# The first normalisation of a fused attention and feed-forward kernel, reordered on all engines

## The reference

```
attention:   4 batches, 8 heads, 576 positions, head width 64
             softmax(q k' / 8 + mask) v       heads 0-3: the last 32 positions
                                              heads 4-7: every 32nd position
feed-forward: rms = sqrt(mean(x*x, axis=-1) + 1e-6);  xn = x / rms * rms_g
             out = (silu(xn @ w_gate) * (xn @ w_val)) @ w_out      width 1536
experts:     8 experts of width 1024, each token goes to the one with the largest logit
             relu(x @ w1[e]) @ w2[e], scaled by the softmax gate
```

## Time and profile before

| what | us |
|---|---|
| median of 3 runs | 873.07 |
| lowest and highest | 871.36 and 874.25 |
| span of the profiled execution | 870.5 |
| TensorE busy | 857.1 (98%) |
| VectorE busy | 520.7 (60%) |
| ScalarE busy | 374.4 (43%) |
| GpSimd busy | 328.4 (38%) |

### The profile page before, as it was taken

One profiled execution on the slowest core, in us unless ns is written; L12 is line 12 of the kernel. 1 busy time (PEld: TensorE's weight loads), 2 busy tenths in 40 slices (PEclk: granted clock), 3 DMA queues, 4 the chain that ended last, 5 costly groups with the idle time before them and its releaser, 6 DMA issues.

```text
span 870.5 us, 15612 instructions
## 1 busy us (share of the span) xinstructions
PE 857.1 (98%) x5233; PEld 736.4 (85%) x5242; DVE 520.7 (60%) x1401; ACT 374.4 (43%) x945; POOL 328.4 (38%) x372
## 2 busy tenths in 40 slices
PE   8999999999999999999999999999999999999997
PEld 5678898888888888899999999988888888888885
DVE  6985555333453335449778763883877457666663
ACT  6966313545464455443321132243356235554442
POOL 3736762344323443356335333170043221222211
PEclk9999999999999999999999999999999999999999
DMA  9983212212223210242121121526265645555531
GB/s 191 289 212 88 61 48 65 84 55 78 53 60 112 52 38 27 71 157 74 42 93 61 61 73 37 210 81 254 97 205 206 241 144 191 184 213 182 192 128 39
DMA packets 77517, 103.40 MB, mean 119 GB/s; under 512 B 38973, under 2 KB 43069, under 8 KB 77312
## 3 DMA queue, kind: packets, MB, share of 16 engines
q1 hardware_dynamic: 73760, 91.16, 33.9%
q0 software_dynamic: 3680, 11.28, 3.7%
HBM read 92.98 MB, written 10.22 MB: 119 GB/s over the span
## 4 chain that ended last, share of the span: by engine, by line
PE 89%; DVE 8%; issue 1%; ACT 1%; POOL 1%; DMA 1%; SPq 0%; DVEq 0%; POOLq 0%; ACTq 0%
PE ps L1243 32%; PE ps L1282 16%; PE ps L1805 13%; PE ps L1790 13%; PE ps L1174 3%; PE ps L1203 2%; PE ps L1815 2%; PE ps L1184 2%; PE ps L1150 2%; PE ps L660 1%; DVE sm L1520 1%; DVE w_lo L2041 1%; DMA qk<-in_k 1%; PE ps L1312 1%; DVE h_lo L1600 1%
## 5 line engine op out<-in xcount | busy, mean ns | idle before, releaser
L1035 POOL TENSOR_TENSOR sm<-sm,rinv 72x288 f32<-72x288 f32 (+1 forms) x51 | 45.5, 893 | 174.2 <-DVE rinv L1531 174.1
L1067 POOL TENSOR_TENSOR out_lo<-out_raw,out_hi 128x512 fp32r<-128x512 f32 x72 | 101.8, 1414 | 5.8
L1589 DVE SCALAR_TENSOR_TENSOR h<-h,ps 128x384 f32<-128x384 f32 x72 | 39.8, 553 | 104.2 <-ACT h L1437 103.3
L1243 PE MATMUL ps<-x_hi,val_hi 128*128 128x384 f32 x288 | 101.1, 351 | 0.0
L1243 PE MATMUL ps<-x_hi,gate_hi 128*128 128x384 f32 x288 | 100.5, 349 | 0.4 <-DVE h L1589 0.4
L1065 POOL CAST out_hi<-out_raw 128x512 fp32r<-128x512 f32 x72 | 50.0, 694 | 135.0 <-DMA out_raw<-in_moe_w_out 135.0
L1441 ACT ACTIVATE h_hi<-h 128x384 fp32r<-128x384 f32 x72 | 37.8, 525 | 138.7 <-DVE h L1595 138.7
L1243 PE MATMUL ps<-x_hi,gate_lo 128*128 128x384 f32 x288 | 97.1, 337 | 0.0
L1243 PE MATMUL ps<-x_hi,val_lo 128*128 128x384 f32 x288 | 96.6, 336 | 0.0
L1243 PE MATMUL ps<-x_lo,val_hi 128*128 128x384 f32 x288 | 96.5, 335 | 0.0
L1243 PE MATMUL ps<-x_lo,gate_hi 128*128 128x384 f32 x288 | 93.9, 336 | 0.0
(11 more groups left out here) (278 smaller groups left out, 1947.5 us busy)
## 6 DMA issues: line engine op xcount, KB each, us to landing
w_raw<-in_moe_w SPq DMA_DIRECT2D x72, 512.0 KB, 4.9
out_raw<-in_moe_w_out SPq DMA_DIRECT2D x72, 256.0 KB, 2.6
x_rows<-y_tiles SPq DMA_DIRECT2D x18, 256.0 KB, 2.7
early_w_raw<-in_moe_w SPq DMA_DIRECT2D x8, 512.0 KB, 7.6
gate_raw<-in_moe_w_gate SPq DMA_DIRECT2D x4, 768.0 KB, 9.1
val_raw<-in_moe_w_val SPq DMA_DIRECT2D x4, 768.0 KB, 10.5
qk<-in_q SPq DMA_DIRECT2D x8, 288.0 KB
qk<-in_k SPq DMA_DIRECT2D x8, 288.0 KB
```

What stands on the lines that cost most here:

```text
L1035: pool.tensor_tensor(s3, s3, rinv[0:n, i, :].unsqueeze(2).to_broadcast([n, 4, c]), ALU.mult).then_inc(s_no, 1)
L1067: pool.tensor_tensor(ol[i][:, :], o_raw[i][:, :], oh[i][:, :].bitcast(f32), ALU.subtract).then_inc(s_ol, 1)
L1243: mm = pe.matmul(ps[:, bank, 0:CH], w[:, i, kk, cols], x[:, kk, :], start=(m == 0), stop=(m == n - 1))
L1589: dve.scalar_tensor_tensor(out=hf[n % 2][:, :], in0=hf[n % 2][:, :], scalar=1.0, in1=ps[:, 0, 0:CH], op0=ALU.add, op1=ALU.mult).then_inc(s ...
```

## The change

The parts are:

1. In GpSimd's loop the normalises of a tick now go ahead of its squares, and the last square of chunk 0 is at tick 15 instead of 16. It is followed by a multiplication of the gain by 0.375, for which GpSimd waits for the load of the gain.
2. Quarter 0 of val is rounded at tick 17 instead of 13, and GpSimd itself then subtracts its two halves (`first_val_lo`).
3. The sums of chunk 0 are split: those of `nr` at tick 16, those of `sq` at tick 17, into two banks, added by VectorE. The mean's factor is in the column of constants `share`.
4. The roots have eight linked operations after the variance instead of eleven and no diagonals: one bit trick, one Newton step and one step of higher order, whose factor 0.375 is in the gain. They are spread by three transposes of a root column read as broadcast. This holds for all chunks.
5. In VectorE's loop the inverts now go ahead of the roots, and normalise and split of x ahead of the mask passes of tick 19.
6. ScalarE splits x in pieces of one, one and two, around the evacuations of tick 19. The exps of groups 18 and 19 move from ticks 18 and 20 to ticks 20 and 21.
7. `first_block` issues block 0 of chunk 0 as hi terms of gate, hi terms of val, lo terms of gate, lo terms of val, one to a tick. The values of tick 20 go behind its first part.
8. The matmuls of constants are 2, 3, 2 and 2 in ticks 16 to 19 instead of 3, 3, 2 and 4. The root spread of chunk 0 goes ahead of those of tick 18.

```diff
-EXPS = {j: SCORE[j] + (0 if j < HEAD - 1 else 1) for j in range(G)}
-INVERT = {j: SCORE[j] + (1 if j < HEAD - 1 else 2 if j < HEAD else 3) for j in range(G)}
+EXPS = {j: SCORE[j] + (0 if j < HEAD - 2 else 2 if j < HEAD else 1) for j in range(G)}
+INVERT = {j: SCORE[j] + (1 if j < HEAD - 2 else 2 if j < HEAD else 3) for j in range(G)}
-SQUARES = {(0, 2): 8, (0, 3): 12, (0, 0): 14, (0, 1): 16}
+SQUARES = {(0, 2): 8, (0, 3): 12, (0, 0): 14, (0, 1): 15}
-SPLIT_V = {0: 13, 1: at(0, 1, 1), 2: at(0, 4, 1), 3: at(0, 7, 1)}
+SPLIT_V = {0: 17, 1: at(0, 1, 1), 2: at(0, 4, 1), 3: at(0, 7, 1)}
...
         def front_pool(pool):
...
             pool.memset(ones[:, :], 1.0).then_inc(s_cst, 1)
+            pool.memset(share[:, :], 1.0 / DM).then_inc(s_cst, 1)
...
                 pool.tensor_tensor(sq[:, :], x, x, ALU.mult).then_inc(s_sq, 1)
                 if kk == ORDER[-1] and c == 0:
+                    pool.wait_ge(s_gain, 16)
+                    pool.tensor_scalar(rms_gain[:, :], rms_gain[:, :], 0.375, None, ALU.mult).then_inc(s_gain38, 1)
                     return
...
+            def first_val_lo():
+                pool.wait_ge(s_wh, SPLIT_NO[1, 0] + 1)
+                for ks in (slice(0, KT // 2), slice(KT // 2, KT)):
+                    pool.tensor_tensor(vl[:, 0, ks, :], v_raw[:, 0, ks, :], vh[:, 0, ks, :].bitcast(f32),
+                                       ALU.subtract).then_inc(s_fv, 1)
...
             for s in range(TICKS):
+                for j in NORM_AT.get(s, []):
+                    normalise(j)
                 if s < EARLY:
                     for c, kk in SQUARES_AT.get(s, []):
                         square(c, kk)
-                for j in NORM_AT.get(s, []):
-                    normalise(j)
                 for val, i in SPLIT_AT.get(s, []):
                     w_hi(val, i)
+                    if (val, i) == (1, 0):
+                        first_val_lo()
...
         def front_pe(pe):
...
-            def sum_squares(c):
-
-                if c:
-                    bank_7_free(("ss", c))
-                else:
-                    pe.wait_ge(s_cst, 3)
-                    pe.wait_ge(s_qe, TURNED_QK[EARLY])
-                pe.wait_ge(s_sq, sq_steps(c + 1))
+            def sum_squares(of, bank, done=s_ssq):
+
                 for t in range(TT):
-                    cols = slice(t * P, (t + 1) * P)
-                    mm = pe.matmul(ps[:, ss_bank(c), t:t + 1], nr[:, cols], ones[:, 0:1], start=True, stop=c > 0)
-                    if c == 0:
-                        mm = pe.matmul(ps[:, ss_bank(c), t:t + 1], sq[:, cols], ones[:, 0:1], start=False, stop=True)
-                mm.then_inc(s_ssq, 1)
+                    mm = pe.matmul(ps[:, bank, t:t + 1], of[:, t * P:(t + 1) * P], share[:, :],
+                                   start=True, stop=True)
+                mm.then_inc(done, 1)
+
+            def first_sums():
+
+                pe.wait_ge(s_cst, 4)
+                pe.wait_ge(s_qe, TURNED_QK[EARLY] - 1)
+                pe.wait_ge(s_sq, sq_steps(1) - 1)
+                sum_squares(nr, ss_bank(0), s_ssp)
 
             def spread_roots(c):
 
                 if c:
                     bank_7_free(("rb", c))
-                pe.wait_ge(s_dg, c + 1)
-                pe.matmul(ps[:, rb_bank(c), 0:CH], ones[:, :], diag[:, :, :].rearrange("p t n -> p (t n)"),
-                          start=True, stop=True).then_inc(s_rb, 1)
+                pe.wait_ge(s_nw, 8 * c + 8)
+                for t in range(TT):
+                    mm = pe.transpose(ps[:, rb_bank(c), t * P:(t + 1) * P], root[:, t:t + 1].to_broadcast([P, P]),
+                                      ident[:, :])
+                mm.then_inc(s_rb, 1)
...
+            def first_block(low, val):
+
+                if not low:
+                    if val:
+                        pe.wait_ge(s_oe, VALUED[EARLY])
+                        pe.wait_ge(s_fv, 2)
+                    else:
+                        pe.wait_ge(s_qe, TURNED_QK[EARLY])
+                        pe.wait_ge(s_wl, 2)
+                wh, wl = (vh, vl) if val else (gh, gl)
+                for kk in range(KT):
+                    for w, x in ((wh, xl),) if low else ((wh, xh), (wl, xh)):
+                        if not val:
+                            pe.wait_ge(s_xl if low else s_xh, kk + 1)
+                        mm = pe.matmul(ps[:, val, 0:CH], w[:, 0, kk, 0:P], x[:, kk, :],
+                                       start=(low == 0 and kk == 0 and w is wh), stop=(low == 1 and kk == KT - 1))
+                if low:
+                    mm.then_inc(s_vp if val else s_g, 1)
...
                 if s == SS[0] + 1:
-                    sum_squares(0)
+                    pe.wait_ge(s_qe, TURNED_QK[EARLY])
+                    pe.wait_ge(s_sq, sq_steps(1))
+                    sum_squares(sq, rb_bank(0))
                 for j in TURN_AT.get(s, []):
                     turn_probs(j)
-                for j in PV_AT.get(s, []):
-                    values(j)
+                if s != EARLY:
+                    for j in PV_AT.get(s, []):
+                        values(j)
                 if s >= EARLY:
                     for key in QK_AT.get(s, []):
                         turn_qk(*key)
+                if s == SS[0]:
+                    first_sums()
+                if s == SPREAD[0]:
+                    spread_roots(0)
                 if s < EARLY:
-                    keep_busy({16: 3, 17: 3, EARLY - 1: 4}.get(s, 2))
+                    keep_busy({17: 3}.get(s, 2))
...
                 if s >= EARLY:
                     c, f, sub, half = step_of(s)
-                    if sub == 0:
+                    if s < EARLY + 4:
+                        first_block(sub, half)
+                    elif sub == 0:
                         gate_product(c, f, half)
...
+                if s == EARLY:
+                    for j in PV_AT.get(s, []):
+                        values(j)
...
         def front_act(act):
...
+                if s == SPREAD[0] + 1:
+                    x_split(0, range(0, 1))
                 for j in TURN_AT.get(s, []):
                     evac_probs(j)
+                if s == SPREAD[0] + 1:
+                    x_split(0, range(1, 2))
                 for j in PV_AT.get(s, []):
                     evac_o(j)
...
                 if s == SPREAD[0] + 1:
-                    x_split(0)
+                    x_split(0, range(2, KT))
                 for j in EXPS_AT.get(s, []):
                     exps(j)
...
             def roots(c):
...
-                if c:
-                    dve.wait_ge(s_dg, c)
+                if c:
+                    dve.wait_ge(s_rb, c)
                 dve.wait_ge(s_ssq, c + 1)
-                dve.tensor_scalar(var[:, :], ps[:, ss_bank(c), 0:TT], 1.0 / DM, 1e-6, ALU.mult, ALU.add).then_inc(s_nv, 1)
+                part = ps[:, ss_bank(c), 0:TT]
+                if c:
+                    dve.tensor_scalar(var[:, :], part, 1e-6, None, ALU.add).then_inc(s_nv, 1)
+                else:
+                    dve.wait_ge(s_part, 1)
+                    dve.tensor_tensor(var[:, :], newt[:, :], ps[:, rb_bank(c), 0:TT], ALU.add).then_inc(s_nv, 1)
                 dve.wait_ge(s_nv, c + 1)
-                link(dve.tensor_scalar(halved[:, :], var[:, :].bitcast(i32), 1, None, ALU.logical_shift_right))
-                link(dve.tensor_scalar(root[:, :].bitcast(i32), halved[:, :], -1.0, 1597463007.0, ALU.mult, ALU.add))
-                for i in range(3):
-                    link(dve.scalar_tensor_tensor(out=newt[:, :], in0=root[:, :], scalar=-0.5, in1=root[:, :],
-                                                  op0=ALU.mult, op1=ALU.mult))
-                    link(dve.tensor_tensor(newt[:, :], newt[:, :], var[:, :], ALU.mult))
-                    link(dve.scalar_tensor_tensor(out=root[:, :], in0=newt[:, :], scalar=1.5, in1=root[:, :],
-                                                  op0=ALU.add, op1=ALU.mult))
-                dve.wait_ge(s_sq, sq_steps(c + 1))
-                dve.tensor_tensor(diag[:, :, :], ident[:, :].unsqueeze(1).to_broadcast([P, TT, P]),
-                                  root[:, :].unsqueeze(2).to_broadcast([P, TT, P]), ALU.mult).then_inc(s_dg, 1)
+                link(dve.tensor_scalar(root[:, :].bitcast(i32), var[:, :].bitcast(i32), -0.5, 1597463007.0,
+                                       ALU.mult, ALU.add))
+
+                link(dve.scalar_tensor_tensor(out=newt[:, :], in0=root[:, :], scalar=-0.5, in1=root[:, :],
+                                              op0=ALU.mult, op1=ALU.mult))
+                link(dve.tensor_tensor(newt[:, :], newt[:, :], var[:, :], ALU.mult))
+                link(dve.scalar_tensor_tensor(out=root[:, :], in0=newt[:, :], scalar=1.5, in1=root[:, :],
+                                              op0=ALU.add, op1=ALU.mult))
+
+                link(dve.tensor_tensor(newt[:, :], root[:, :], root[:, :], ALU.mult))
```

(67 more changed lines are left out.)

1 line of the change is left out of this document (removed).

## The result

The changed kernel takes 876.74 us in the median of 17 executions (875.19 to 879.68). The kernel before, on the same chip, takes 872.37 (869.37 to 879.51, 17 executions). The ratio is 1.005, 95% interval 1.0036 to 1.0064: slower by 4.4 us where the forecast said 1.8 more and its low-clock rival 4.4 more. The profiled execution has a span of 876.6 us (870.5 before) and a mean granted clock of 0.991. In every kernel here the time of an execution is its span and 1.7 to 1.8 us, so the profiled execution of the changed kernel (878.3) lies 1.6 above the median.

A forecast was written before the change was run, and what follows sets the result against it. From the first feed-forward product TensorE's work bounds the kernel (98% busy); before it, timelines show an 8 us root chain. Front +2.5, clock +0.8, chunks -1.5 gave +1.8 on 873.07: 874.9, 8-in-10 range 868.8 to 877.0.

The forecast's parts named there:

- low-clock rival: First block, 52 to 59 us: TensorE stays at half clock for some 7 us; +4.4, so 877.5; chance 0.14.
- the links: Chunk 0's roots on VectorE: GpSimd's normalise, cast and two subtractions hold the links; root ready at R + 6.7 = 52.1.
- The idle time: TensorE ahead of chunk 0's root spread: stands there from 47.4 on and waits 4.7 us.
- Free roots: Chunk 0's roots: links pass beside GpSimd, root at 47.3; with the chunks -4.0, so 869.0; chance 0.26.
- the chunks: Root spreads of chunks 1 to 5: 0.30 saved, five times, -1.5 us, bounds 0 and -2.5.
- the fourth case: Later root spreads: transposes of a broadcast operand save nothing in the chunks; +3.3, so 876.4; chance 0.07.
- so I take +0.8, between 0 and 1.7: Front, after TensorE's wait for the root: cost of the clock falling to the 1.2 GHz level, +0.8 us.
- under 1 somewhere in 50 to 56: Sign expected in the front: TensorE's clock drops below 1 at some point from 50 to 56 us.
- is partly waiting for x_hi: First block after the root: TensorE's next work partly waits for x_hi, the reason given for a clock cost of +0.8.
- the front without the clock: Spread, x and first block of chunk 0: the state of 54.92 is reached at 57.45, +2.5 us.
- Ticks 13 to 16: Chunk 0: normalises ahead of squares remove a 0.49 wait; score 17 at 43.65, sq sums end at 44.8.
- a chain gets one link through for each GpSimd instruction: VectorE beside GpSimd: dependent short SBUF operations advance one link per GpSimd instruction, about 0.5, 1.4 and twice 1.9 us.

The follow-up runs named there:

- the fillers: The changed kernel with 20 more matmuls of constants on TensorE directly ahead of the first root spread: 874.02 us, ratio 1.0015.
- roots ahead of invert 16: The changed kernel with the roots put ahead of invert 16 again in VectorE's loop, all else as changed: 871.53 us, ratio 0.9986.
- GpSimd's wait: The changed kernel with GpSimd waiting for the eighth link of the first roots before it casts quarter 0 of val: 871.24 us, ratio 0.9982.
- part 4 alone: The kernel before with only the eight root links, 0.375 in the gain and three-transpose spread, in all chunks: 871.96 us, ratio 0.9987.
- the old block order: The changed kernel with GpSimd waiting for the first roots, and block 0 in its order of before: 871.22 us, ratio 0.9993.

## Why the prediction was right and wrong

**Right: the links.** Forecast: held by normalise, cast and each subtraction, root 6.7 behind the reciprocal. Measured: the reciprocal ends at 46.44, the last link at 53.06, 6.6. The split among the links was not as forecast: link 1 lasted through normalise and cast together (2.08, where 0.5 and then 1.4 stood), and link 2 went free; the sum is the same. The idle time was put at 4.7 and was 4.30. That the scalar_tensor_tensor link is held too was left open; 1.73 at 50.55 shows that it is. The Trainium skill (SBUF — State Buffer, "SBUF: two separate sides") has the same exclusion, and the trace agrees: 1.65 and 1.73 for 0.16. Free roots, at 0.26, were refuted by this row.

**Right: the chunks.** 0.28 at each spread for 0.30, and transposes of a broadcast column at no extra price: the fourth case falls.

**Wrong: the clock.** The step "so I take +0.8, between 0 and 1.7" is the term that was mis-sized: it measured at least 2.7 (876.74 against 874.02 with the fillers), by the estimate above up to 4.2. I had the fall right and its end wrong. The forecast's sign that the clock is "under 1 somewhere in 50 to 56" was met, but it stayed at 0.50 to about 65, with TensorE busy for 5.00 of 5.00 us in 55 to 60. The reason on record was that what TensorE does next "is partly waiting for x_hi", so that half speed would hide in a wait. There was no such wait: from 53.11 to the values at 60.33 TensorE's timeline shows no idle time, the small groups at half speed fill the time to 57.27, and the hi terms follow at half speed too. Nor did a row say that work brings the clock back soon: the earlier trace rows show 0.50 with TensorE busy for 2.00 of 2.00. The rival *Low clock through the whole first block* named that very point, still 0.50 when the val hi terms start (they started at 62.48), priced it at +4.4, and got 0.14; it reckoned with some 7 us at half, and the stretch was 13.6 (51.2 to 64.9), the last 11.8 of it with work. The Trainium skill's rule that counted for it (TensorE: Matmul & The Clock Gate, "Part 4: PE-mode transpose") is not settled here. With the same transposes and no long wait the clock stayed at 1.00 (roots ahead of invert 16, and GpSimd's wait), so transposes alone did not bring the fall; but part 4 alone lost its clock among scores, transposes and values with hardly a wait.

**Nearly right: the front without the clock.** The medians give 1.6 for the change with fillers, but the kernel before loses some clock in its own median. Executions of both at a mean clock of 0.998 or 0.999 have medians of 874.0 and 871.0, so the change with fillers costs 3.0. With the 1.4 that the chunks give back that is 4.4 in the front; 1.5 of it are the fillers that ran on behind the root. Some 2.9 are left, by estimate, where the forecast had 2.5. Two things in it were not forecast. The step "Ticks 13 to 16" costed the normalise ahead of the squares from tick 13 on, but the diff changes that order at tick 8 too, where it moved a cast onto an `rsum`: 0.8 in the positions, 0.7 when undone. And it put score 17 at 43.65 and the end of the `sq` sums near 44.8; they came at 44.85 and 46.1. I had the lock in hand and applied it to one place only. The second is the waits of 0.53 and 0.90 for xT, where the working had no wait; both stand where the new order puts a turn right behind what ScalarE must still evacuate. How much of them would remain with an early root was not separated, though the 0.90 stayed with GpSimd's wait.

**The range** of 868.8 to 877.0 holds 876.74, at its upper end, and that is luck. It was built on 873.07, a median of three, and the kernel before took 872.37 this time; as a change, the range ended at +3.9 and 4.4 lies beyond. The forecast called its own +1.8 no measurable change and gave a clear slowdown 0.23; a clear slowdown came. The sign was right, the size was of the rival.

## What to carry to other kernels

When a reorder moves a long GpSimd instruction, list every place where it moves one, and in each the short VectorE operations with SBUF operands that will stand beside it, in a chain above all; a wait put on GpSimd until the chain is over cost less than it gave here (876.74 to 871.24), since its result was due late. Price a wait of TensorE of some microseconds as the wait and, behind it, the work at half clock (here 11.8 us of it behind a wait of 4.30), unless matmuls of constants can stand in it. When a kernel's executions fall into groups, compare executions of the same mean clock before believing a median, and compare kernels of different chips by their ratios.

## What the runs showed that I had not expected

The clock of the front falls without a wait to speak of: in the kernel with part 4 alone, where the longest wait between 15 and 60 us was 0.48, and only in half of the executions of that one program, at 4 to 5 us. Why it fell there is open. Six matmuls of constants (128x512) over four ticks removed that group (none in 8 executions). The lock between the engines holds GpSimd as well: a sum of 1.00 took 1.86 beside VectorE's subtraction, and in the kernel with GpSimd's wait the first x_lo took 1.86 beside `val_lo`, where one free of it took 0.55. (The 0.94 in the expectation for the old block order is the mean of four; the longest is 1.86, the shortest 0.55.) The forecast's rule that a chain gets one link through for each GpSimd instruction is rough: one link lasted through two instructions (2.08 at 46.55), and one went through in the gap between two (0.16 at 48.66).
